# Decays for the other partition half copied by ScalarE instead of multiplied into place by TensorE

## Time and profile before

| | |
|---|---|
| median of 3 runs | 1189.07 us (1188.3 to 1198.45) |
| profiled execution | 1192.24 us, span 1190.4 us |
| TensorE matmul (PE) | 1056.8 us busy, 89% of the span, 24816 matmuls and as many weight loads |
| VectorE (DVE) | 538.6 us, 45% |
| ScalarE (ACT) | 383.1 us, 32% |
| GpSimd (POOL) | 325.8 us, 27% |
| mean granted TensorE clock | 0.965 |

### The profile page before, as it was taken

How to read it: one execution, slowest core, us unless ns; L and a number is a source line. 1 busy time by engine, 2 the same in 40 slices (tenths; PEclk the granted TensorE clock), 3 DMA queues, 4 the chain that set the end, 5 groups by cost and what they waited for, 6 DMA issues and landing times. The chain is left out here.

```text
span 1190.4 us, 54426 instructions
## 1 busy us (share of the span) xinstructions
PE 1056.8 (89%) x24816; PEld 786.9 (66%) x24816; DVE 538.6 (45%) x1152; ACT 383.1 (32%) x1021; POOL 325.8 (27%) x588
## 2 busy tenths in 40 slices
PE   4777777899999898899999898799999897899978
PEld 4766677766766676666667677666666686655556
DVE  5444544334334766333334586514334675210274
ACT  2332332222112454322212355432112453310155
POOL 4544454223222433122223343212322320000000
PEclk9898998799999999899999999999999998999989
DMA  6222332312312222112121132211121111000000
GB/s 200 60 85 80 97 85 79 118 55 67 93 39 60 65 75 62 54 27 62 40 59 55 50 85 74 53 33 55 41 61 39 47 53 32 26 1 1 1 12 23
DMA packets 47940, 68.57 MB, mean 58 GB/s; under 512 B 19680, under 2 KB 34784, under 8 KB 47712
## 3 DMA queue, kind: packets, MB, share of 16 engines
q1 hardware_dynamic: 47712, 65.08, 18.8%
HBM read 57.19 MB, written 7.86 MB: 55 GB/s over the span
## 5 line engine op out<-in xcount | busy, mean ns | idle before, releaser
L486 POOL TENSOR_TENSOR QI<-R,consts 128x256 f32<-128x256 f32 x240 | 174.2, 736 | 476.4 <-DVE R L655 440.8
L655 DVE COPY R<-PB 128x512 f32<-128x512 f32 x147 | 101.0, 687 | 188.4 <-PE PB L919 186.3
L548 ACT COPY R<-PB 128x512 f32<-128x512 f32 x147 | 86.6, 589 | 230.5 <-PE PB L919 228.6
L911 PEld LDWEIGHTS PB<-R 64*64 64x64 f32 x5376 | 103.0, 140 | 68.3 <-issue 54.3
L911 PE MATMUL PB<-R 64*64 64x64 f32 x5376 | 124.6, 230 | 25.2 <-issue 10.9
L1144 PE MATMUL PB<-uf,W 128*128 128x384 f32 x320 | 112.0, 496 | 1.4 <-ACT ur L599 1.4
L1171 PE MATMUL PB<-work,W 128*128 128x384 f32 x320 | 108.0, 491 | 2.5 <-DVE work L830 2.5
L1144 PEld LDWEIGHTS PB<-uf,W 128*128 128x128 f32 x320 | 58.0, 190 | 46.7 <-issue 12.8
L919 PE MATMUL PB<-R,QI 64*64 64x64 f32 x3072 | 79.6, 224 | 9.1 <-issue 8.7
L1171 PEld LDWEIGHTS PB<-work,W 128*128 128x128 f32 x320 | 59.2, 190 | 42.1 <-issue 2.9
L830 DVE TENSOR_SCALAR work<-PB 128x384 f32<-128x384 f32 x40 | 22.3, 558 | 127.1 <-PE PB L1149 74.6
(11 more groups left out here) (138 smaller groups left out, 1935.8 us busy)
## 6 DMA issues: line engine op xcount, KB each, us to landing
EA<-ea_dram SPq DMA_DIRECT2D x48, 498.0 KB, 3.5
LA<-la_dram SPq DMA_DIRECT2D x48, 384.0 KB, 3.5
VT<-vt_dram SPq DMA_DIRECT2D x48, 80.0 KB, 1.9
x_mid_dram<-XO SPq DMA_DIRECT2D x192, 20.0 KB, 1.9
xs<-x_mid_dram SPq DMA_DIRECT2D x24, 160.0 KB, 2.8
out_dram<-work SPq DMA_DIRECT2D x24, 160.0 KB, 2.0
W<-w_dram SPq DMA_DIRECT2D x1, 1600.0 KB, 8.1
W<-w_dram SPq DMA_DIRECT2D x1, 1280.0 KB, 8.8
```

Source lines behind the costliest of these rows:

```text
L486: nc.gpsimd.tensor_tensor(QI[j][:].rearrange("p (u g t) -> p u g t", u=2, g=2), src.rearrange("p u (g t) -> p u g t", g=2), eye3.unsqueeze ...
L548: freed(nc.scalar.copy(tile[:, 8 * C:16 * C], PB[PLACE[group, i][0]][:, 1, :]), group, i)
L655: freed(nc.vector.tensor_copy(tile[:, 0:8 * C], PB[PLACE[group, i][0]][:, 0, :]), group, i)
L911: mm = nc.tensor.matmul(out[half(m1), u, col:col + C], left, right, start=True, stop=True)
```

## The change

Part 1 of `PT` no longer has data of its own in the bank. The four products L877 are left out, and ScalarE makes part 1 from the transposed decays of L873: one copy of 64 partitions x 80 columns for each half, read from half `p` of the bank and written to half `1 - p` of `PT`. ScalarE's copies for B3 are four instead of three, and the count in `drains_of` goes from 2 to 3 for the member `s1`.

```diff
-        ops = {"U": 1, "o2": 1, "X": 1, "o3": 1, "s2": 1, "s1": 2, "s3": 2, "ST": 1, "o1": 2}
+        ops = {"U": 1, "o2": 1, "X": 1, "o3": 1, "s2": 1, "s1": 3, "s3": 2, "ST": 1, "o1": 2}
...
                 dst = at(PT, n)[:].rearrange("p (w g d) -> p w g d", w=3, g=2)
-                freed(nc.scalar.copy(dst[:, 0:3:2],
-                                     ps[:, 1, 0:4 * C].rearrange("p (g u c) -> p u g c", g=2, u=2)[:, :, :, 0:D]),
-                      "B3", i)
-                freed(nc.scalar.copy(dst[:, 1], ps[:, 1, 4 * C:4 * C + 2 * D].rearrange("p (g d) -> p g d", g=2)),
-                      "B3", i)
+                src = ps[:, 1, 0:4 * C].rearrange("p (g u c) -> p u g c", g=2, u=2)[:, :, :, 0:D]
+                freed(nc.scalar.copy(dst[:, 0:3:2], src), "B3", i)
+                for p in range(2):
+                    freed(nc.scalar.copy(dst[half(1 - p), 1], src[half(p), 1]), "B3", i)
...
                 for g in range(2):
-                    nc.tensor.transpose(out[:, 1, g * P:(g + 1) * P], at(Pf, n)[:, g * P:(g + 1) * P], ident)
-                for g in range(2):
-                    for p in range(2):
-                        x = 2 * g + p
-                        mm = nc.tensor.matmul(out[half(1 - p), 1, 4 * C + g * D:4 * C + (g + 1) * D],
-                                              at(Pf, n)[feat(1), x * C:x * C + C], eye[feat(1), 0:D],
-                                              start=True, stop=True)
+                    mm = nc.tensor.transpose(out[:, 1, g * P:(g + 1) * P], at(Pf, n)[:, g * P:(g + 1) * P], ident)
                 return mm
```

## The result

The changed kernel's median is 1180.76 us over 15 runs, that of the kernel before 1192.18 us over as many. The ratio is 0.992, interval 0.9891 to 0.995: 6 to 13 us faster where 16 were forecast. Both programs scatter from one execution to the next, by 20 us before and 14 after; one run of the changed kernel, 1654.8 us at a clock of 0.559, is left out of the ratio and of this scatter.

A forecast was written before the change was run, and what follows sets the result against it. The prediction took instruction delivery to bound the first 222 us and TensorE's work the stretches with mixing. Savings of 4.25 + 10.5 + 1.7 = 16.4 us gave about 1173 us, range 1165 to 1182.

The forecast's parts named there:

- The stages beside attention: Nine B3s beside attention: savings less the delays at two of them, 1.7 us saved, bounds -1 and +3.
- The stretches with mixing, 10.5 us: B3s beside mixing, TensorE's work setting the pace: 0.56 or 0.36 us saved each, 10.5 us, bounds 5.2 and 11.1.
- Where C1 follows: B3s followed by C1: the change to small tiles stays, so at most 0.2 us is saved.
- The first 222 us, 4.25 us: Recurrence alone, paced by instruction delivery: 272 fewer instructions at 4.0 us per 256 save 4.25 us, bounds 0 and 5.8.
- My sign against this reading: Recurrence alone: packets coming closer than 4.0 us apart, or stalls moving, would show the delivery reading wrong.
- The rival of a lower clock: TensorE, with less to do between waits, is granted 1.2 GHz more often; result within 1%, chance 0.05.
- The rival built on that rule: Instruction delivery is hidden, so the first stage hangs on the bank chain: 19.9 us saved, 1169.2 us, chance 0.10.
- ScalarE's copy: Part 1 of B3 as two 64 x 80 copies: the extra copy priced at 0.19 to 0.24 us.
- B3's time: B3 is full when the last L873 ends, 0.34 us earlier; the last copy ends 0.10 to 0.15 earlier.
- The two B3s at wide scores: B3s at 486 and 762, one slot of banks: the extra copy delays C1, 0.2 us lost each.
- the rival with ScalarE's copy on the path: Release of B3's banks: the extra copy costs 0.24 us at all 48, 11.5 us slower, 1200.6 us, chance 0.05.
- The rival of waits beside mixing: Beside mixing, waits for banks or `work` take half the saving: 9.5 us saved in all, 1179.6 us, chance 0.17.

The follow-up runs named there:

- the one again: The changed kernel with no edit, timed and profiled a second time against the kernel before: ratio 0.9921.
- the three with no-operations: Changed kernel with no-operations added on TensorE's queue (16 per B3, 256 or 128 at the start), which never reached the chip: 0.9898, 0.988, 0.9895 to the kernel before.
- 32 increments: Changed kernel with 32 increments of a spare semaphore at the start of TensorE's queue: ratio 0.985 to the kernel before.

## Why the prediction was wrong

The direction was right and the size was not: 16.4 us forecast, 6 to 13 measured. Five traces of the changed kernel's work (the first, the one again and the three with no-operations) and two of the kernel before give the stages on the mean. The recurrence alone is 3.2 us shorter, where 4.25 was forecast. The three mixing stages are 3.7, 1.7 and -0.9 us shorter, 4.5 in all, where their 20 B3s, 14 at 0.56 and 6 at 0.36, make 10.0. The stages beside attention scatter too much with the granted clock to test their 1.7.

**The stretches with mixing, 10.5 us, are the step that failed.** The price of each B3 was right to 0.01 us, 0.56 and 0.36. (Where C1 follows, 0.07 us came of the 0.2: from the first load of L872 to that of C1's second product are 426.19 - 425.31 = 0.88 us, against 438.34 - 437.39 = 0.95.) What failed is the sentence that execution sets the pace there, and so that instruction delivery needs counting only in the first stage. I read that from the mean distance of the packets, 5.9 us. A mean hides that the portions are uneven: one in full-array work takes 8 to 9 us (834.8 to 843.7 in the third stage after), one that lies wholly in A1 to A3 takes 2.2, less than the 3.0 to 3.4 us in which the next becomes ready. Whether TensorE then stops depends on where the borders lie, and I removed 16 instructions from a period without asking where they would then lie. TensorE's idle time at "issue" in the three mixing stages was 1.2 and 0.9 us in the two traces before and is 4.5 and 5.7 in the first two after. The third stage shows it alone: 2.96 us saved, and 3.3 given back, of which 2.8 are the three stops; with borders elsewhere 2.9 us of the saving remain.

**The first 222 us, 4.25 us.** The mechanism is supported: the packets fell by 3 and the stage was 221.5 and 216.5 us for 223.25 and 221.7 before, 3.5 us on the means of two profiles each (3.2 with all five after, 216.5 to 221.5), inside the scatter. My sign against this reading, that the stalls move, was no sign: where borders lie is fixed by the count, so they had to move when instructions went. But 4.0 us for each 256 instructions is not the whole law of this stage. 32 increments, forecast at +0.5 us, came with 209.62 us and a clock of 0.96 instead of 0.92 (0.90 in the second profile). Why the place of the borders is worth so much here is open; that stops lower the granted clock, and the clock lengthens the executions between stops, would fit but was argued only. The rival of a lower clock did not come: 0.91 before.

**The rule weighed against the trace.** "Runtime: NRT & Kernel Launch", section "Instruction fetch mechanics", in the Trainium skill says that fetching blocks of 256 is hidden. These runs disagree: moving the blocks by 32 instructions moved the third mixing stage by 3 us, and TensorE's stops end some 1.4 us after a packet lands. The rival built on that rule (faster still, because the first stage hangs on waits) did not come true.

**ScalarE's copy was mis-sized and B3's time was not.** ScalarE's timeline after, at the B3 whose loads are shown above:

```profile
257.19 0.58 ACT L551 COPY BKf<-PB 128x512 f32<-128x512 f32 x1 [0.50 <-PE PB L872]
257.68 0.30 ACT L558 COPY PT<-PB 128x160 f32<-128x160 f32 x1
258.00 0.46 ACT L560 COPY PT<-PB 64x80 f32<-64x80 f32 x2
```

From the first load of L872 to the start of `BKf` are 257.19 - 256.67 = 0.52 us; before, 262.62 - 261.73 = 0.89 (the first time from that timeline, the second from the earlier trace rows). B3 is full 0.37 us earlier, forecast 0.34. But the copies last from 257.19 to 258.46, 1.27 us, against 438.29 to 439.20, 0.91 us, in the earlier trace rows: the swap costs 0.36 us, not 0.19 to 0.24. A copy of 64 partitions takes 0.22 us, near the 0.24 of one of 128 partitions with as many columns, but the first starts 0.32 us after L558 where L560 started 0.19 after L557. So parts 0 and 2 and `BKf` come earlier, and the last copy and `DEN` do not, where I had 0.10 to 0.15.

**The two B3s at wide scores** came out as forecast in sign, near in size. The second after:

```profile
473.08 0.58 ACT L551 COPY BKf<-PB 128x512 f32<-128x512 f32 x1
...
473.89 0.46 ACT L560 COPY PT<-PB 64x80 f32<-64x80 f32 x2
```

```profile
474.40 0.69 PE L904 MATMUL PB<-R 64*64 64x64 f32 x32 [0.95 <-ACT PT L560]
```

From the first matmul of L872, at 472.41, to C1 are 1.99 us. Before, L873's first matmul was at 486.25 and C1 at 488.00, 1.75 us: 0.24 us lost in place of 0.2. So the rival with ScalarE's copy on the path is real at these two of 48 places. The runs with the products left in put the copy's whole price at about 3 us, each with an interval that reaches 0; where the other 2.5 us of it lie is open.

**The rival of waits beside mixing** gave the right size (9.5 us) for a wrong reason: no bank and no `work` became late. PE's idle time behind a semaphore is 2.24, 0.84 and 0.75 us in the three mixing stages, before and after alike; what grew is at "issue".

## What to carry to other kernels

Where a long unrolled queue has stretches of many short instructions, count instructions between its stalls in the timeline; if the number is constant, a stall's place is set by what stands ahead of it, and any edit that changes a count moves it. Then look in the DMA view for packets of the instruction queue beside the stalls. Before crediting or blaming an edit of 1%, move the borders alone, by a few instructions where the engine idles anyway. Here the change with borders moved by 32 instructions and part 1 on GpSimd gave 0.9795 and 0.9839, the fastest version.

## What was not expected of the hardware

A semaphore increment on TensorE's queue takes 0.151 us, against 0.014 us from load to load in small tiles. 32 of them, costing nothing where they stand, went with 0.985 for 0.990 in the changed kernel and with 1.010 for 1 in the kernel before. TensorE did not go on before the next packet of its instructions had been there for 1.0 to 1.65 us, at all but 3 of the 859 stops counted above. And since one period of this loop is near 1024 instructions, a border can meet the same products period after period.
